# Moving half of a weight's rounding behind the first exponential, and starting row tiles at unit 13

## The reference

```
w = softmax(weight over its 7 taps)                       # 8 heads, each for 24 channels
x = causal convolution of x with w                        # 7 taps per channel
h = x @ w_in1                                             # 192 -> 2048
g = (a0 + a1 h + a2 h^2 + a3 h^3) / (1 + |b0||h| + |b1| h^2 + 1e-6)
x = g @ w_out1                                            # 2048 -> 192   (layer 1)
h = x @ w_in2                                             # 192 -> 2048
out = (s * relu(h)^2 + b) @ w_out2                        # 2048 -> 192   (layer 2)
```

## Time and profile before

| | us |
|---|---|
| Median of 3 runs (1236.22 to 1237.65) | 1236.22 |
| Profiled execution, own time | 1235.03 |
| Profiled execution, span of its instructions | 1233.2 |
| PE busy (99% of the span) | 1216.2 |
| DVE busy (88%) | 1081.7 |
| ACT busy (88%) | 1081.0 |
| POOL busy (31%) | 382.9 |

### The profile page before, as it was taken

One profiled execution on the slowest core, in us unless ns is written; L12 is line 12 of the kernel. 1 busy time (PEld: TensorE's weight loads), 2 busy tenths in 40 slices (PEclk: granted clock), 3 DMA queues, 4 the chain that ended last, 5 costly groups with the idle time before them and its releaser, 6 DMA issues.

```text
span 1233.2 us, 25178 instructions
## 1 busy us (share of the span) xinstructions
PE 1216.2 (99%) x10722; PEld 1083.8 (88%) x10722; DVE 1081.7 (88%) x957; ACT 1081.0 (88%) x1128; POOL 382.9 (31%) x196
## 2 busy tenths in 40 slices
PE   8998999999999999999999999999999999999999
PEld 5666889898988999998999998899898998999898
DVE  7998799998999999998999989999899998888810
ACT  7998898989889898899988999898998899888843
POOL 3444333224223242232422333223323333232200
PEclk9999999999999999999999999999999999999999
DMA  7200000001000100001000000001000000000000
GB/s 229 62 2 24 2 1 14 2 14 27 14 1 2 40 1 15 1 1 40 1 14 2 14 28 1 14 2 27 13 15 1 1 15 1 15 1 14 2 14 14
DMA packets 14832, 21.63 MB, mean 18 GB/s; under 512 B 1792, under 2 KB 9984, under 8 KB 14592
## 3 DMA queue, kind: packets, MB, share of 16 engines
q1 hardware_dynamic: 14576, 20.01, 5.5%
q10 hardware_dynamic: 144, 0.01, 0.0%
HBM read 13.72 MB, written 6.29 MB: 16 GB/s over the span
## 4 chain that ended last, share of the span: by engine, by line
PE 91%; DVE 5%; issue 1%; ACT 1%; DMA 1%; SPq 0%; POOL 0%; DVEq 0%; ACTq 0%; POOLq 0%
PE o L663 23%; PE h L641 20%; PE h L635 19%; PE o L647 13%; PE o_tail L653 8%; PE o L503 3%; DVE work L1120 1%; DVE work L1088 1%; DVE work L1127 1%; DVE work L1094 1%; DVE work L1091 1%; DMA work<-in_moe_w_out_dram 1%; PE h L495 1%; PE h L496 1%; PE h L485 1%
## 5 line engine op out<-in xcount | busy, mean ns | idle before, releaser
L443 POOL TENSOR_TENSOR gl<-work,gh 128x1024 fp32r<-128x1024 f32 x126 | 304.0, 2413 | 487.6 <-ACT gh L872 485.8
L663 PE MATMUL o<-v,work 64*128 64x192 f32 x3584 | 332.1, 322 | 0.0
L663 PEld LDWEIGHTS o<-v,work 64*128 64x128 f32 x3584 | 310.4, 186 | 12.0
L862 ACT ACTIVATE work<-h,coef 128x1024 f32<-128x1024 f32 x128 | 154.1, 1204 | 87.9 <-PE h L635 83.1
L1088 DVE SCALAR_TENSOR_TENSOR work<-work,coef,h 128x1024 f32<-128x1024 f32 x128 | 163.7, 1279 | 74.7 <-ACT work L863 73.3
L1131 DVE SCALAR_TENSOR_TENSOR work<-work,coef 128x1024 f32<-128x1024 f32 x128 | 164.4, 1285 | 4.5
L1094 DVE SCALAR_TENSOR_TENSOR work<-work,coef,h 128x1024 f32<-128x1024 f32 x128 | 163.9, 1281 | 4.5
L1120 DVE SCALAR_TENSOR_TENSOR work<-work,coef 128x1024 f32<-128x1024 f32 x128 | 166.4, 1300 | 0.8 <-ACT work L867 0.8
L1127 DVE SCALAR_TENSOR_TENSOR work<-work 128x1024 f32<-128x1024 f32 x128 | 156.8, 1225 | 4.4
L899 ACT ACTIVATE work<-h 128x1024 f32<-128x1024 f32 x128 | 129.8, 1014 | 32.6 <-PE h L496 32.3
L954 ACT ACTIVATE work<-work,coef 128x1024 f32<-128x1024 f32 x128 | 146.9, 1148 | 11.3 <-POOL gl L443 9.3
(11 more groups left out here) (142 smaller groups left out, 2711.2 us busy)
## 6 DMA issues: line engine op xcount, KB each, us to landing
out_dram<-y_out SPq DMA_DIRECT2D x32, 192.0 KB, 2.1
xt<-in_x_main_dram SPq DMA_DIRECT2D x7, 518.0 KB, 4.6
xt_tail<-in_x_tail_dram SPq DMA_DIRECT2D x8, 259.0 KB, 4.6
work<-in_moe_w_out_dram SPq DMA_DIRECT2D x2, 768.0 KB, 9.1
v<-in_moe_w_out_dram SPq DMA_DIRECT2D x1, 1536.0 KB, 7.4
raw_w_tail_late<-in_moe_w_in_dram SPq DMA_DIRECT2D x4, 256.0 KB, 6.6
work<-in_moe_w_in_dram SPq DMA_DIRECT2D x2, 512.0 KB, 6.2
xt<-in_x_main_dram SPq DMA_DIRECT2D x2, 259.0 KB, 6.4
```

The lines of the kernel that those rows point to most:

```text
L443: nc.gpsimd.tensor_tensor(gl[:, j % 2, :], r_buf[j % 2], gh[:, j % 2, :].bitcast(F32), ALU.subtract).then_inc(gl_ready, 1)
L663: last = pe.matmul(o2[:, bank, c, 0:D], g2[buf_out][rows, col:col + P], v2[rows, f, :], start=(f == 0 and c == 0 and turn == 0), stop=(f = ...
```

## The change

Three things change. ScalarE rounds the second half of v1 and piece 2 of w1 behind unit 0's exponential: the first no longer ahead of unit 0, the second no longer between unit 1's first steps and unit 0's Abs. The low part of that half of v1 is made by GpSimd, behind `t3_done` of unit 0 and ahead of the low parts of w1's piece 2. The counts waited for follow the new order. And TensorE uses the row form from unit 13 (`ROWS_FROM = SKEW + OUT2_LAG`) in place of unit 16. All `isinstance` tests on loop numbers are dropped.

```diff
+    ROWS_FROM = SKEW + OUT2_LAG
...
-        def by_rows(t):
-            return not isinstance(t, int) or 2 <= t < TILES
+        def by_rows(n):
+            return ROWS_FROM <= n < NU
...
         # GpSimd
-            low_of_w1(PIECES[1], 7)
+            low_of_w1(PIECES[1], 5)
             pool.wait_ge(w_ready, 2)
             pool.wait_ge(t3_done, 1)
+            f = V1_HALF[1]
+            pool.wait_ge(w_hi_ready, 7)
+            nc.gpsimd.tensor_tensor(v1_lo[:, f, :], raw_v1[:, f, 0:P], v1_hi[:, f, :].bitcast(F32),
+                                    ALU.subtract).then_inc(v1_lo_ready, 1)
+            pool.wait_ge(w_hi_ready, 8)
+            nc.gpsimd.tensor_tensor(v1_tail[:, f, 1, :], raw_v1[:, f, P:D], v1_tail[:, f, 0, :].bitcast(F32),
+                                    ALU.subtract).then_inc(v1_lo_ready, 1)
...
         # TensorE, product_of_layer_1
-                    high, low = {1: (2, 4), 2: (8, 6), 4: (10, 9), 6: (10, 10)}[j]
+                    high, low = {1: (2, 4), 2: (6, 6), 4: (10, 9), 6: (10, 10)}[j]
         # TensorE, unit_by_rows
-                since = n - 2 * UNITS
+                since = n - ROWS_FROM
...
                 if k_out == 0:
+                    pe.wait_ge(conv_copied, 3)
+                    pe.wait_ge(v2_loaded, 16)
...
+                if m == UNITS // 2:
+                    pe.wait_ge(w_hi_ready, 14)
+                    pe.wait_ge(w_lo_ready, 18)
...
         # ScalarE
-            for half in range(2):
+            def high_of_v1(half):
                 f = V1_HALF[half]
                 act.wait_ge(v1_loaded[half], 16)
                 high_of_weight(v1_hi[:, f, :], raw_v1[:, f, 0:P])
                 high_of_weight(v1_tail[:, f, 0, :], raw_v1[:, f, P:D])
+            high_of_v1(0)
...
                         first_steps(1, h2_flat, num_buf[1], q_buf[1])
-                        high_of_w1_main(2)
-                        high_of_w1_tail(2)
...
                         exponential(n, buf)
+                    if n == 0:
+                        high_of_v1(1)
+                        high_of_w1_main(2)
+                        high_of_w1_tail(2)
...
         # VectorE
-            for half in range(2):
-                f = V1_HALF[half]
-                low_of_weight(v1_lo[:, f, :], raw_v1[:, f, 0:P], v1_hi[:, f, :], 3 + 2 * half)
-                low_of_weight(v1_tail[:, f, 1, :], raw_v1[:, f, P:D], v1_tail[:, f, 0, :], 4 + 2 * half)
+            f = V1_HALF[0]
+            low_of_weight(v1_lo[:, f, :], raw_v1[:, f, 0:P], v1_hi[:, f, :], 3)
+            low_of_weight(v1_tail[:, f, 1, :], raw_v1[:, f, P:D], v1_tail[:, f, 0, :], 4)
```

More of the change, by code:

```diff
@@ L21, in counted @@
 def counted(count):
-    return max(count, 0) if isinstance(count, int) else count
+    return max(count, 0)
 def conv_rational_relu2_kernel(nc, x_main, x_tail, weight, w_in1, w_out1, a, b, w_in2, w_out2, s, b2, out):
@@ L72, in pair_exists @@
     def pair_exists(i):
-        return not isinstance(i, int) or i < TPB
+        return i < TPB
     def tokens(i, batch):
@@ L225, in in_h2 @@
         def in_h2(n):
-            return isinstance(n, int) and n < EARLY and n % 2 == 1
+            return n < EARLY and n % 2 == 1
         def is_unit_1(n):
-            return isinstance(n, int) and n == 1
+            return n == 1
         def ahead(n):
-            return isinstance(n, int) and 1 <= n <= EARLY
+            return 1 <= n <= EARLY
         def cast_early(n):
-            return isinstance(n, int) and 0 <= n <= EARLY - 3
+            return 0 <= n <= EARLY - 3
         def late_exponential(n):
-            return not isinstance(n, int) or n >= EARLY - 1
+            return n >= EARLY - 1
         def by_vector(n):
-            return isinstance(n, int) and n >= NU - 2
-        def by_rows(t):
-            return not isinstance(t, int) or 2 <= t < TILES
+            return n >= NU - 2
+        def by_rows(n):
+            return ROWS_FROM <= n < NU
         def later_pair(i):
-            return not isinstance(i, int) or i > 0
+            return i > 0
         def is_end(n):
-            return isinstance(n, int) and n == NU
+            return n == NU
         def unit(n):
-            return not isinstance(n, int) or 0 <= n < NU
+            return 0 <= n < NU
         def tile(t):
-            return not isinstance(t, int) or 0 <= t < TILES
+            return 0 <= t < TILES
         def is_last(t):
-            return isinstance(t, int) and t == TILES - 1
+            return t == TILES - 1
         def first(t):
-            return isinstance(t, int) and t == 0
+            return t == 0
         def second(t):
-            return isinstance(t, int) and t == 1
+            return t == 1
         def main_steps(pair):
-            return 0 if isinstance(pair, int) and pair == 0 else (pair - 1) * TAPS
+            return 0 if pair == 0 else (pair - 1) * TAPS
         def tail_steps(pair):
-            return TAPS if isinstance(pair, int) and pair == 0 else pair * TAPS
+            return TAPS if pair == 0 else pair * TAPS
         def run(phase):
@@ L316, in load_x @@
             def load_x(pair):
-                sp.wait_ge(conv_summed, 2 if isinstance(pair, int) and pair == 1 else 5)
+                sp.wait_ge(conv_summed, 2 if pair == 1 else 5)
                 sp.wait_ge(tail_step, counted(tail_steps(pair - 1)))
@@ L394, in phase @@
                     n = n0 + j
-                    if isinstance(n, int) and n == 3:
+                    if n == 3:
                         c = LAST_HALVES[1]
@@ L400, in phase @@
                         low_of_weight(w1_tail_lo[:, c], raw_tail(c), w1_tail_hi[:, c], 10)
-                    if isinstance(n, int) and n in W2_LOW_AT:
+                    if n in W2_LOW_AT:
                         rows, half, part = W2_LOW_AT[n]
@@ L581, in product_of_layer_1 @@
                 if first(t) and j in (1, 2, 4, 6):
-                    high, low = {1: (2, 4), 2: (8, 6), 4: (10, 9), 6: (10, 10)}[j]
+                    high, low = {1: (2, 4), 2: (6, 6), 4: (10, 9), 6: (10, 10)}[j]
                     pe.wait_ge(w_hi_ready, high)
                     pe.wait_ge(w_lo_ready, low)
-                two_buffers = isinstance(n, int) and n <= EARLY
+                two_buffers = n <= EARLY
                 pe.wait_ge(t3_done, counted(n - 1 if two_buffers else n))
@@ L758, in phase @@
                     t2 = t + (j - SKEW) // UNITS
-                    if by_rows(t):
+                    if by_rows(n):
                         unit_by_rows(n, j, t, parity, m, k2, t2)
                         continue
-                    early = isinstance(n, int) and n < EARLY
-                    if unit(n) and not (isinstance(n, int) and n <= EARLY):
+                    early = n < EARLY
+                    if unit(n) and not (n <= EARLY):
                         product_of_layer_1(n, j, t, parity)
@@ L793, in phase @@
                             pe.wait_ge(w_lo_ready, 14)
-                        if isinstance(m, int) and m == UNITS // 2:
+                        if m == UNITS // 2:
                             pe.wait_ge(w_hi_ready, 14)
@@ L874, in convolved @@
             def convolved(pair):
-                if isinstance(pair, int) and pair == 1:
+                if pair == 1:
                     act.wait_ge(conv_copied, 2)
@@ L970, in phase @@
                         copy_of_conv(conv[:, 1, :], 0)
-                    if isinstance(n, int) and n in W2_HIGH_AT:
+                    if n in W2_HIGH_AT:
                         rows, half = W2_HIGH_AT[n]
@@ L978, in phase @@
                             high_of_weight(w2_tail_hi[:, W2_HALF[half]], raw_w2_tail[half])
-                    for k in TAIL_DIAG_AT.get(n, ()) if isinstance(n, int) else ():
+                    for k in TAIL_DIAG_AT.get(n, ()):
                         act.wait_ge(w_lo_ready, 12)
```

## The result

The changed kernel takes 1243.17 us (median of 6 runs, 1242.49 to 1244.05) against 1235.83 (6 runs of before): ratio 1.0061, 95% interval 1.005 to 1.0072. It is 7.3 us slower, beyond the upper end of the predicted range (1240.2). Its profiled execution has a span of 1242.0 against 1233.2.

The account below looks back on a forecast made before the run. Bound by VectorE's chain in the start-up, then by TensorE's time per unit. Start-up +2.8 and row tiles -1.16 gave +1.6 us on a median of 1236.22, so 1237.9, range 1234.2 to 1240.2.

Parts of the forecast that it names:

- Rounding moved behind the exponential: ScalarE's start-up: unit 0 starts 1.28 us earlier, its Newton step 2.15 earlier; casts paid back, leaving 0.4 gain at unit 2.
- The low part made by GpSimd: Start-up: GpSimd and VectorE take turns on two-SBUF-input instructions, so unit 3 starts later; +2.8 us taken.
- Queues it is moved past: SP's load queue: v2 lands at 42.6 to 43.5 us, in time for TensorE's column sum; nothing added.
- the deadline of 43.7: Latest column sum start on TensorE without delaying unit 3's Newton step: 41.07 us, shifted by 2.65.
- Slower: v2 lands late: Rival, chance 0.17: between product 4 and unit 0's second product, column sum becomes the bound; +2 us taken, 1239.9.
- Row tiles from unit 13: Units 13 to 15 on TensorE: three units take 27.44 us in place of 28.60, saving 1.16.
- A shift arrives unchanged: From start-up to 115.21 us: any delay of units 2 and 3 on VectorE's chain arrives there in full.
- the main case: Whole kernel: GpSimd and VectorE take turns, v2 in time, row tiles save; 1236.9 to 1238.9 us, chance 0.54.

Follow-up runs that it names:

- e1: Kernel before with only the row tiles changed, from unit 13; start-up as before: 1234.56 us, ratio 0.9988.
- e8: e1 plus 21 unread matmuls in TensorE's four idle stretches between 93 and 115 us: 1232.67 us, ratio 0.9982.
- e7: Changed kernel with the low part of v1's second half left out (zeros) and GpSimd's two subtracts shrunk to 8 elements: 1238.41 us, ratio 1.0024.
- e2: Changed kernel's start-up alone, with row tiles from unit 16 as in the kernel before: 1243.73 us, ratio 1.0065.
- e6: Changed kernel with v1's low part by VectorE and w1's piece 2 rounded before unit 0's Abs; only v1's casts stay moved: 1243.99 us, ratio 1.0072.
- e9: e6 with SP loading v2 ahead of its wait for v1's low part: 1236.01 us, ratio 1.0006.
- e5: Changed kernel with unread matmuls behind unit 2's taps and product 4, and the column sum behind product 5: 1240.22 us, ratio 1.0041.
- e10: e7 plus unread matmuls behind unit 2's taps and product 4, and the column sum behind product 5: 1236.92 us, ratio 1.0014.
- e3: Changed kernel with TensorE's column sum over v2 one unit later, behind product 5 in place of product 4: 1242.08 us, ratio 1.005.
- e4: Changed kernel with unread matmuls in TensorE's idle stretches ahead of product 4 and of the wait for v2: 1240.96 us, ratio 1.0039.
- e11: Changed kernel with the 21 unread matmuls of e8 added between products 11 and 13: 1241.07 us, ratio 1.0045.

## Why the prediction was wrong

By its own steps:

- *Rounding moved behind the exponential.* The order of waits was right, the gain was partly luck. The Newton step came at 26.54 (26.07 predicted), 1.68 earlier than before. Half of that is the earlier start of unit 0 on VectorE (19.25 in place of 20.07, where 18.79 was predicted), and e1 and e8 start at 19.24 and 19.10 with no cast moved: the 1.28 were read off one execution in which v1 landed late. ScalarE pays back: unit 2's second activation starts at 30.78 (30.3). With GpSimd's part small (e7) unit 2 starts at 31.64, ScalarE being last (31.6).
- *The low part made by GpSimd.* The mechanism was right, the size low by 0.7: unit 3 at 42.90, 3.48 later than before, +2.8 taken. Some 0.5 of the difference is the start itself (VectorE's unit 0 at 19.25, not 18.79, since unit 0's product was ready only at 16.9), most of the rest the second meeting, where gl went first and held L1141 for 3.46.
- *Queues it is moved past.* This step failed: "It fits, by 0.2 to 1.1: nothing added, if the clock is full". v2 was issued at 35.77 (35.2) and landed at 44.85 (42.6 to 43.5): 9.1 us with w2's loads just ahead of it, not 7.4. The sum started at 44.99, past the deadline of 43.7, which is 44.55 with the shift of 3.48 that was measured: 0.44 too late. And the clock was not full: 8.42 in place of 5.56, 2.86 more. 0.44 + 2.86 = 3.3 is what unit 3's Newton step lost over unit 3's start (6.79 - 3.48). The clock is the larger part, and it does not need a late landing: in e2 the sum starts within 0.1 of its deadline (41.07, moved by the 2.61 by which unit 3 is later there) and in e7 0.8 ahead of it, and in both the Newton step is late. The late gl then met it, 1.26 more: 8.05 at unit 5 (62.89 against 54.84 before).
- *Slower: v2 lands late.* This rival, at 0.17, is what happened. Its place was right. Its point of decision, a start after 43.7, holds at full clock alone, as e2 and e7 show. Its price was too low: I gave it the 3 us of half clock that stand before, and here it lasted from 44.99 to past 50 (0.50 until 50, 0.74 from 50 to 52), and the meeting with gl behind it was left out. Measured it is 0.44 + 2.86 + 1.26 = 4.6, where I took 2.
- *Row tiles from unit 13.* Right: 152.29 - 125.03 = 27.26 in place of 28.60 for three units; 1.2 us by e1's median.
- *A shift arrives unchanged.* Right up to 111.51 (+8.21); behind it the clock adds 1.6 in the profiles. In the medians 8.2 - 1.2 = 7.0 stands against 7.3 measured.

What let it be wrong is that I kept the clock out of the main case and asked only whether v2 would be in time, when a start in time (42.6 to 43.5) at half clock was 0.4 to 1.3 over by my own numbers. And forecasting a margin of 0.2 to 1.1 us on a landing whose bounds I had put at 42.6 and 45.4 did not justify three times the weight for "in time".

The causes do not add up, and I leave it at this. A late v2 with no meeting ahead of unit 3 costs 8.0 us (e6 against e9, medians). The changed kernel loses 8.6 against e1; with the column sum later and the clock kept up it still loses 5.7 (e5 against e1), and with v1's part of GpSimd gone as well 2.4 are left (e10 against e1; 3.2 by the ratios). Why v2 took 9.1 us to land is open: w2's loads just ahead of it are the likely reason, but e3 with the same spacing took 10.8.

## What to carry to other kernels

When a step moves to another engine, follow the semaphore it raises into every queue that waits for it: here SP issues in order, and in e6 a wait that had moved from 19 to 33 us held back a load that had nothing to do with it (8 us, e6 against e9). In these traces work given to GpSimd cost VectorE nothing beside instructions with a tensor in PSUM, and whole instructions beside those with all tensors in SBUF. Count what already fits beside the former, since what doesn't fit pushes the next piece onto a busy stretch. A late transfer was paid twice where TensorE waited for it, in the wait (0.44 us past what was free) and in the clock behind it (2.86). And an earlier start read off one profile may be that execution's slow load: compare the same row in a second execution first.

## What the runs showed that I had not expected

In e1 three idle stretches of 0.9 to 1.8 us, ending at 94.9, 99.2 and 101.8, were followed by a half clock (0.86 as a mean of 95 to 105 us); with unread matmuls in them it was 1.00 (e8). The lengths alone do not decide it: ahead of the same three products TensorE was idle for 1.02, 1.13 and 1.82 in before's profiled execution, which kept 1.00, and for 1.02, 1.17 and 1.82 in the changed kernel's, which fell to the half clock. A 128x8 subtract on GpSimd took 1.32 us when it was issued beside a VectorE instruction with both tensors in SBUF, and 0.21 right after: small size does not avoid the wait. The same 1.5 MB load took 6.4 us to land with none of w2's loads issued ahead of it (e9), 7.3 to 7.5 with the last of them issued over 5 us earlier (before, e1, e8), 8.0 and 8.1 at 2 us (e7, e10), 8.5 to 9.1 and once 10.8 at 1.2 us (the changed kernel, e2, e4, e5, e11; e3), and 12.2 right behind them (e6).
